# One expert's row weights and row numbers copied one expert earlier in a mixture-of-experts stage

## The reference, cut to what matters

```python
def _moe2_ref(x, w_gate, w1, w2, capacity):        # x (1152, 512), w1 (8, 512, 1024), w2 (8, 1024, 512)
    logits = x @ w_gate
    expert_idx = np.argmax(logits, axis=1)
    ...
    gate_w = probs[np.arange(N), expert_idx]
    # rows are placed in order into their expert's slots, up to capacity (288)
    ...
    h = np.maximum(np.einsum('ecd,edf->ecf', disp, w1), 0.0)
    y = np.einsum('ecf,efd->ecd', h, w2)
    for i in range(N):
        if keep[i]:
            out[i] = gate_w[i] * y[expert_idx[i], pos[i]]
```

## Time and profile before

| | us |
|---|---|
| median of 3 executions | 666.29 |
| lowest, highest | 663.3, 668.44 |
| the profiled execution | 663.3 |
| its span (first to last instruction) | 661.5 |

### The profile page before, as it was taken

One profiled execution on the slowest core, in us unless ns is written; L12 is line 12 of the kernel. 1 busy time (PEld: TensorE's weight loads), 2 busy tenths in 40 slices (PEclk: granted clock), 3 DMA queues, 4 the chain that ended last, 5 costly groups with the idle time before them and its releaser, 6 DMA issues.

```text
span 661.5 us, 13482 instructions
## 1 busy us (share of the span) xinstructions
PE 609.7 (92%) x4302; PEld 547.1 (83%) x4302; DVE 526.0 (80%) x1017; ACT 439.5 (66%) x728; POOL 289.8 (44%) x294
## 2 busy tenths in 40 slices
PE   4668798799999999999999999999888999999995
PEld 3455697698797897997988988989678999999995
DVE  5999999897989979989989986015629878788761
ACT  2667377769779679688597696835528655667540
POOL 0376457648467377466575474830600110011111
PEclk9988599899999999999999999999999999999999
DMA  5875600000000000000000000051388766767400
GB/s 180 353 324 192 250 5 5 17 14 5 25 5 5 25 5 5 25 9 1 28 4 16 0 0 18 1 194 46 128 312 306 278 213 216 288 199 271 147 14 19
DMA packets 17792, 68.62 MB, mean 104 GB/s; under 512 B 1998, under 2 KB 6606, under 8 KB 15056
## 3 DMA queue, kind: packets, MB, share of 16 engines
q1 hardware_dynamic: 16000, 63.27, 25.9%
q0 software_dynamic: 1744, 4.73, 2.0%
HBM read 54.33 MB, written 14.45 MB: 104 GB/s over the span
## 4 chain that ended last, share of the span: by engine, by line
PE 64%; ACT 14%; POOL 9%; issue 7%; DVE 3%; DMA 2%; POOLq 0%; ACTq 0%; SPq 0%; DVEq 0%
PE p_a L1281 7%; PE p_o L1243 7%; PE p_b L1281 5%; PE p_s L1205 5%; PE p_b L1303 4%; PE p_t L1222 3%; PE p_b L1305 3%; PE p_s L1498 3%; PE p_b L1304 3%; POOL arena L678 3%; PE p_t L1498 3%; PE p_t L1475 3%; PE p_s L1475 3%; ACT arena L843 2%; POOL w_out_lo L717 2%
## 5 line engine op out<-in xcount | busy, mean ns | idle before, releaser
L374 DVE MAX8 top<-arena 128x8 f32<-128x576 f32 x288 | 201.2, 746 | 7.4 <-ACT arena L843 7.4
L377 DVE MATCH_REPLACE8 arena<-top,arena 128x576 f32<-128x576 f32 x216 | 158.7, 742 | 0.0
L678 POOL TENSOR_TENSOR arena<-arena,pen 128x576 f32<-128x576 f32 x72 | 100.7, 1421 | 57.3 <-ACT pen L850 57.3
L1243 PEld LDWEIGHTS p_o<-arena,probsT 128*128 128x128 f32 (+1 forms) x720 | 84.2, 188 | 14.2 <-ACT probsT L870 8.2
L1243 PE MATMUL p_o<-arena,probsT 128*128 128x65 f32 (+1 forms) x720 | 89.6, 270 | 6.9 <-ACT probsT L870 5.2
L870 ACT COPY probsT<-p_t 128x384 f32<-128x384 f32 x108 | 51.3, 480 | 52.1 <-PE p_t L1222 51.9
L1303 PE MATMUL p_b<-w_out_lo,g_hi 128*128 128x512 f32 x144 | 62.9, 437 | 5.6 <-DVE g_lo L404 3.7
L1222 PE MATMUL p_t<-ident,arena 128*128 128x128 f32 x324 | 55.7, 283 | 12.6 <-ACT arena L862 12.6
L1281 PE MATMUL p_a<-xT,wff 128*128 128x128 f32 x512 | 65.9, 283 | 0.0
L1281 PE MATMUL p_b<-xT,wff 128*128 128x128 f32 x512 | 64.3, 279 | 0.0
L1281 PEld LDWEIGHTS p_a<-xT,wff 128*128 128x128 f32 x512 | 60.8, 195 | 2.8 <-issue 2.4
(11 more groups left out here) (187 smaller groups left out, 1309.5 us busy)
## 6 DMA issues: line engine op xcount, KB each, us to landing
arena<-in_w SPq DMA_DIRECT2D x8, 2048.0 KB, 9.3
wff<-in_w SPq DMA_DIRECT2D x8, 2048.0 KB, 9.6
slot_rows<-y_now SPq DMA_DIRECT2D x1, 4626.0 KB, 15.8
wff<-in_w_out SPq DMA_DIRECT2D x1, 4096.0 KB, 12.2
wff<-in_w_in SPq DMA_DIRECT2D x1, 4096.0 KB, 22.9
wff<-slot_rows SPq DMA_DIRECT2D x8, 385.5 KB, 3.9
arena<-in_vones SPq DMA_DIRECT2D x2, 1300.0 KB, 16.8
q_sb<-in_q SPq DMA_DIRECT2D x36, 64.0 KB, 2.0
```

What stands on the lines that cost most here:

```text
L374: nc.vector.max(best, src).then_inc(top_step, 1)
L377: nc.vector.match_replace(work[:, a, :], best, src, LOWEST).then_inc(top_step, 1)
L678: nc.gpsimd.tensor_tensor(s_sb[:, t, :], s_sb[:, t, :], pen[:, t % 2, :], ALU.subtract).then_inc(masked, 1)
L1243: last = mm(p_o[q, lo:lo + n], probsT[:, g % 2, P * c + q.start:P * c + q.stop], vones[b][:, p, at:at + n], start=(k == 0), stop=(k == PAI ...
```

## The change

`keep` of expert E is taken out of expert E, where it stood behind `scale_rows`, and `keep` of expert E + 1 is put into expert E, between `low_x(E + 1)` and `low_w1(E + 1)`. The call ahead of the loop stays.

```diff
@@ in expert(E, j, turn, n, more) of the vector engine
                     low_w2(E, j, 0)
                 else:
                     scale_rows(E - 1, 1 - j, turn - 1 + j, n)
-                    keep(E, j, turn, n)
                 sum_unit(E, 2, n)
                 low_he(E, 1, n)
@@
                 if more:
                     low_x(E + 1, n)
+                    keep(E + 1, 1 - j, turn + j, n)
                     low_w1(E + 1, 1 - j, range(4) if begin else (2, 3))
                     low_w2(E + 1, 1 - j, 0)
                 sum_unit(E, 4, n)
```

## The result

| | before | after |
|---|---|---|
| median, us | 666.85 (4 runs) | 687.12 (4 runs) |
| lowest to highest | 663.3 to 668.44 | 684.84 to 689.58 |
| ratio, 95% interval | | 1.0312 (1.0248 to 1.0378) |
| profiled execution, and its span | 663.3, 661.5 | 684.15, 682.4 |

The kernel is 3.1% slower, 20.3 us by the medians and 20.9 us by the spans. The forecast was 2.0% (679.4 us), with a range that ended at 686. The direction and the main mechanism were right, the size too small.

What follows compares the result with a forecast made beforehand. TensorE sets the 20.4 us period of each middle expert. Removed copies 0, added copies 0.1 and the wait 5 x 2.6 = 13.0 sum to +13.1 us, on the median 666.29 making 679.4 us; range 671.5 to 686.

Steps and rivals of the forecast that it cites:

- the new wait: VectorE at keep's new place waits for the scatter of E-1, issued in the same expert; cost 13.0 us over five experts.
- the removed and the moved copies: Two small VectorE copies per expert: removal gains 0, at most 0.9 us; at the new place +0.1 us, in expert 0.
- the slack of 1.2 us at sum 5: At turn_back(E,1) TensorE needs sum 5, which VectorE has ready 1.25 us ahead, say 1.2 with the handover.
- rival (a): At keep's new place no wait decides, as scatters come through before the slot: 665.5 to 666.4 us; chance 0.08.
- the push of VectorE: Delay of VectorE's work behind keep, per waiting expert: 4.8 us with traffic as it was, less 1.0 relief, 3.8 us.
- five windows: Experts 1 to 5, from low_w1's start to the scatter's last packet: 4.4, 5.0, 4.0, 4.5, 4.5 us, mean 4.5.
- The relief by the rows' move: Row load now follows the w2 load, so 0.39 MB leaves the engines before w1 and the scatters: 1.0 us less push.
- Rival (c): At the scatter wait, no relief or worse, w1 getting further ahead: 18 us and more, 684 to 690 us; chance 0.18.
- theory A: For w1 in four DMAs: packets served in turn, some four already taken ahead; scatter lands 2 to 4 us earlier.
- the law: For the five waiting experts, TensorE loses five times (VectorE's push less 1.2 us of slack at sum 5).

Runs made afterwards that it cites:

- e3: Changed kernel, but SP issues the w1 load of E+2 only when the scatter of E-1 has landed: 665.27 us, ratio 1.0.
- e1: Against the kernel before, only keep's copy of the weights moves to the new place; the numbers and the scatter wait stay: 664.82 us, ratio 0.9994.
- e2: Against the kernel before, both copies move, numbers into a spare tile, copied on behind the scatter wait at the old place: 665.25 us, ratio 0.999.
- e6: Changed kernel with keep(E + 1) moved later, behind the last low_w2: 665.87 us, ratio 0.9998.
- e7: Changed kernel with keep(E + 1) one step earlier, ahead of low_x: 695.4 us, ratio 1.0428.
- e4: Changed kernel with each w1 load issued as four DMAs of 4 KB per partition instead of one of 16 KB: 675.41 us, ratio 1.0133.
- e5: Changed kernel with keep(E + 1) one step later, behind low_w1 and low_w2(0), ahead of sum 4: 669.1 us, ratio 1.0051.

## Why the prediction was wrong in size

**What held.** That the new wait names the scatter of E-1; that five experts wait and expert 6 does not; that the load of w1 is what makes the scatter late (e3); that the removed and the moved copies are worth nothing beyond 0.1 us in expert 0 (e1, e2, e6); that VectorE catches up before the next wait and TensorE does not, so that it repeats; that TensorE idles for sum 4 and again for sum 5 (in experts 1, 4 and 5; in 2 and 3 only for sum 4); the slack of 1.2 us at sum 5 (the table above). The rule quoted from the Trainium skill ("DMA: Bandwidth & Descriptors", section "Anatomy of one DMA — SWDGE (gpsimd) path", about 2.0 us plus the bytes over the rate) fits a scatter that has the engines to itself, 2.7 to 2.9 us in e3 against the estimate of 2.5, and misses the one beside a 2 MB load, about 8 us, by over 5 us; rival (a), which it supported, did not come.

**The step that failed** is the push of VectorE, "Push: 4.8 - 1.0 = 3.8 us". It measured 5.05 us, and the 1.25 us have four parts:

- The landing was read too early, 0.2 us. Two of my five windows showed 62 and 63 packets of the scatter where the others had 64, and I took their ends for the end. The missing ones came later. Queue 0 of the kernel before, from 550.4 to 551.0 and from 590.8 to 591.5:

```profile
q0 software_dynamic: 2, 0.00, 0.2%
...
q0 software_dynamic: 1, 0.00, 0.1%
```

  The last packets were at 550.8 and 591.4, not 550.2 and 590.5, and the mean from low_w1 to them is 4.7 us, not 4.5. The wait asks for all 32 increments of the two halves, so the very last packet is its end, however small.
- The relief by the rows' move was taken as 1.0 us. The landing came 8.4 - 7.95 = 0.5 us earlier in the changed kernel (0.5 us). The sign was right (e1 against e2 shows up to 1.0), but the relief went to the wrong transfer: the w1 load, forecast to land 9.0 us after its issue, lands after 8.2, 9.0, 8.2, 8.1 and 8.4 us, against 9.6 to 10.0 before, while the scatter keeps its 8 us in experts 1, 3 and 5 and gains only in 2 and 4 (9.3 and 9.1 before, 8.0 and 7.8 after).
- From the last packet to VectorE's first copy I took 0.2 us, from the kernel's end, where the engines have nothing else to do. In the five experts it was 0.4 to 0.5, in expert 2 1.2, mean 0.6 (0.4 us).
- The copies took 0.25 us behind a wait, not the 0.13 of two copies that run on from other work (0.1 us).

5 x 1.25 is 6.2 us, all of it passed on, since the slack was already used up. Then two terms that had no place in my sum: TensorE's lower clock in experts 2 and 3, 1.0 us, in the traced execution, and 0.6 us before the first wait, where the two executions differ ahead of anything that was moved. 13.1 + 6.2 + 1.0 + 0.6 = 20.9, the difference of the spans. Rival (c), "no relief or worse", gave 18 us and more, 684 to 690 us, and the measured 687.1 lies in it. Its reason (w1 gets further ahead and the scatter stays at its old landing) is in part what was seen: the second half's first packet comes 5.0 to 5.1 us after its start in the changed kernel and 4.7 to 4.8 in the one before, and in three experts of five the landing has not moved. But the number is no proof of that reason alone, since most of the missing push has other sources: the landing read too early, the time behind the last packet, and the copies.

**How the range came out too narrow.** I held 1.0 us of relief for the middle between none and all, but the landing, the time behind the last packet and the copies were all counted from below, and each is multiplied by five behind a slack that has been used up. The miss of the range is small: the executions at the higher clock, 684.2 to 684.9 us, lie inside it, and the two at the lower clock lift the median to 687.1.

Left open: why expert 2's scatter took 1.2 us from its last packet to VectorE, twice or more the others' time (it does so again in e7, but takes 0.5 us in e4 and e5); what decides whether the clock falls around an idle time of about 2.4 us or not; and whether the pieces that pass in front of the scatter had been taken up ahead of it, as theory A has it, which no run shows directly.

## What to carry to other kernels

A wait on a buffer's last reader gets a whole period younger when the write is moved one stage earlier, even if nothing in its line of code changes: turn + j looked like a renaming, and it named the scatter whose second half had started 3.5 us before. The small scatter beside the 2 MB load took about as long as the load (8 us, against 3 alone), so ask at each such wait which bulk load is issued in the same stretch; moving the wait by a few steps (e6), holding the load back until the scatter is through (e3), or taking the data out through a spare tile (e2) each removed all of it. And count a wait's end to the last of its packets, and every delay behind an exhausted slack in full.

## What the runs showed of the hardware that was not expected

- The second half of a scatter, 0.16 MB, got no packet through for 3.3 us while 1.03 MB of a load in the other queue passed in 16 KB pieces, though that load was issued only 1.2 us before the scatter's issue was over (issue at 521.92, end at 523.17). With 4 KB pieces it took 6.1 us from its start to its last packet instead of 8, and the kernel before with the same pieces is no slower (ratio 0.9985).
- Holding the w1 load back by 3.4 us cost nothing (665.27 us): it landed after 8.8 us and 1.5 us ahead of its use.
- An idle time of TensorE can cost more than itself: in e7, where it idled 3.6 to 4.0 us once in each of experts 2 to 4, its mean granted clock was 0.87 over these experts, and the five periods lost 30.5 us where the law gives 24.8.
